# One attention and two mixture-of-experts layers on one core: weight loads reordered, two tile preparations moved from ScalarE to VectorE, and filler matmuls added

## The reference, cut to what matters

```
x = softmax(0.125 * mean_pool2(q) @ k.T) @ v       # 2 batches, 8 heads, 1152 keys, 576 pooled queries, width 64
x = x as (1152 tokens, 512)
layer 0: e = argmax(x @ w_gate); g = softmax weight of e     # 8 experts, at most 288 tokens each
         x = g * (relu(x @ w1[e]) @ w2[e])                   # w1[e] is 512x1024, w2[e] is 1024x512
layer 1: tokens with x @ w_skip > 0 only:
         x = x + g * (relu(x @ w1[e]) @ w2[e])               # own weights; other tokens are kept
```

## Time and profile before

| | us |
|---|---|
| median of 3 runs | 679.82 (678.68 to 680.38) |
| the profiled execution, its own time | 677.86 |
| its span, first to last instruction | 676.1 |
| PE busy | 585.8 (87%) |
| DVE, ACT, POOL busy | 308.4, 281.8, 182.1 |
| PE's share of the chain that ended last | 80% |

### The profile page before, as it was taken

The page is one execution under the profiler, slowest core; times in us unless marked ns, Lnnn a source line. Parts: engine busy times, 40 slices in busy tenths (PEclk is TensorE's granted clock), DMA queues, the critical chain, the costliest instruction groups (busy, mean ns, idle before and its releaser), DMA issues.

```text
span 676.1 us, 11932 instructions
## 1 busy us (share of the span) xinstructions
PE 585.8 (87%) x3420; PEld 329.2 (49%) x3421; DVE 308.4 (46%) x651; ACT 281.8 (42%) x454; POOL 182.1 (27%) x166
## 2 busy tenths in 40 slices
PE   3759999999999999938999999996569846699994
PEld 3547778777777777533333333332523212233331
DVE  5326665756665666570266629555611101022222
ACT  4525565666565655324333444410045030444410
POOL 5183562618081900001111112111012202022222
PEclk9878999999999999958999999999579959799998
DMA  4786536371717160079398059670471854951111
GB/s 105 157 294 132 139 71 142 73 157 35 157 43 149 53 248 19 1 281 383 113 394 357 31 184 413 246 274 20 170 271 48 312 227 127 405 178 51 53 50 40
DMA packets 42633, 111.56 MB, mean 165 GB/s; under 512 B 16020, under 2 KB 16020, under 8 KB 41536
## 3 DMA queue, kind: packets, MB, share of 16 engines
q1 hardware_dynamic: 38528, 99.03, 45.6%
q0 software_dynamic: 4080, 12.22, 5.4%
HBM read 102.68 MB, written 12.06 MB: 170 GB/s over the span
## 4 chain that ended last, share of the span: by engine, by line
PE 80%; DVE 5%; DMA 4%; issue 3%; ACT 2%; POOL 2%; SPq 1%; DVEq 0%; ACTq 0%; POOLq 0%
PE psum L887 39%; PE psum L680 13%; PE psum L694 10%; PE psum L728 8%; PE psum L874 4%; PE psum L756 2%; DMA qraw<-in_q_dram 2%; DMA w1ring<-in_moe_w_dram 2%; ACT wright L313 1%; PE psum L740 1%; PE psum L724 1%; PE psum L852 1%; POOL KT L328 1%; PE psum L889 1%; SPq L387 1%
## 5 line engine op out<-in xcount | busy, mean ns | idle before, releaser
L887 PE MATMUL psum<-w1ring,XT 128*64 x304 | 142.7, 625 | 29.0 <-ACT wright L313 23.6
L889 PE MATMUL psum<-wright,XT 128*64 128x512 f32 x304 | 142.7, 625 | 0.0
L887 PE MATMUL psum<-w2ring,HT 128*64 x304 | 134.5, 595 | 3.2 <-DVE wright L313 3.1
L889 PE MATMUL psum<-wright,HT 128*64 128x512 f32 x304 | 134.5, 595 | 0.0
L1131 DVE TENSOR_SCALAR_CACHE_REDUCE probs<-psum 128x1152 f32<-128x1152 f32 x72 | 97.6, 1357 | 74.2 <-PE psum L680 74.2
L680 PE MATMUL psum<-KT,QT 128*128 128x384 f32 x480 | 106.5, 362 | 19.6 <-DVE KT L1238 9.8
L971 ACT ACTIVATE probs<-probs,nmax 128x1152 f32<-128x1152 f32 x72 | 90.7, 1260 | 48.0 <-DVE probs L1131 48.0
L313 ACT COPY wright<-w1ring 128x1024 f32 x76 | 74.6, 1058 | 61.1 <-DMA w1ring<-in_moe_w_dram 35.0
L680 PEld LDWEIGHTS psum<-KT,QT 128*128 128x128 f32 x480 | 84.6, 197 | 31.3 <-issue 16.6
L887 PEld LDWEIGHTS psum<-w1ring,XT 128*64 128x64 f32 x304 | 42.0, 144 | 114.9 <-issue 114.9
L694 PE MATMUL psum<-ident,probs 128*128 128x128 f32 x648 | 83.1, 277 | 3.3 <-ACT probs L971 2.8
(11 more groups left out here) (160 smaller groups left out, 563.8 us busy)
## 6 DMA issues: line engine op xcount, KB each, us to landing
w1ring<-in_moe_w_dram SPq DMA_DIRECT2D x64, 512.0 KB, 9.2
w2ring<-in_moe_w_dram SPq DMA_DIRECT2D x64, 512.0 KB, 6.6
qraw<-in_q_dram SPq DMA_DIRECT2D x30, 288.0 KB, 7.0
kraw<-in_k_dram SPq DMA_DIRECT2D x14, 576.0 KB, 7.1
V<-in_v_dram SPq DMA_DIRECT2D x8, 576.0 KB, 3.9
moe_in<-zero SPq DMA_DIRECT2D x9, 256.0 KB, 3.0
wnext<-in_next_w_dram SPq DMA_DIRECT2D x1, 2304.0 KB, 16.5
out_dram<-moe_in SPq DMA_DIRECT2D x1, 2304.0 KB, 9.7
```

The lines of the kernel that those rows point to most:

```text
L887: pe.matmul(psum[0:GRAIN, b, :], lhs[:, c * P:c * P + GRAIN], left, start=first, stop=last, skip_group_check=True)
L889: return pe.matmul(psum[GRAIN:P, b, :], lhs[:, c * P + GRAIN:(c + 1) * P], wright[k][:, cols], start=first, stop=last, skip_group_check=True)
```

## The change

Six edits:

1. SP waits for layer 0's first gather before it loads any w2. Inside a layer w1 of expert a + 2 is asked for before w2 of expert a, and w1 of expert 4 ahead of the loop. All first seven matrices of layer 1 are loaded during layer 0.
2. The right half of w1 for the tiles 0 and 1 is filled by DVE: for tile 0 right after the tables, ahead of the rest of the routing, and for tile 1 behind w2's first fill, once hidden(0) is done. ACT fills from tile 2 on.
3. Layer 0's last y is copied by ACT into a tile of its own (`ylast`), from which PE and POOL read.
4. PE's loop passes over the missing tiles first, directly behind step 0, and then runs the tiles in order.
5. 22 filler matmuls (ident by ident, 128x128) on PE before the first scores, and 8 in each layer, behind the gate placement, once `rows_in` is there. Their result is not read.
6. `turn_y` and PE's logits use other PSUM banks.

```diff
@@ SP
+            sp.wait_ge(x_loaded_[0], 16)
             load_matrix(SECOND, 0, 0)
             load_matrix(SECOND, 0, 1)
-            sp.wait_ge(x_loaded_[0], 16)
+            load_matrix(FIRST, 0, 3)
             load_matrix(SECOND, 0, 2)
-            load_matrix(FIRST, 0, 3)
...
-            def other_experts(m):
-                with sp.Fori(RINGS[1], E - 1) as a:
-                    load_second(m, a, m, a - RINGS[1])
-                    load_first(m, a + 1, m, a - RINGS[1])
-                load_second(m, E - 1, m, E - 1 - RINGS[1])
+            def middle_experts(m):
+                load_first(m, RINGS[0], m, 0)
+                with sp.Fori(RINGS[1], E - 2) as a:
+                    load_first(m, a + 2, m, a - 2)
+                    load_second(m, a, m, a - RINGS[1])
             sp.wait_ge(tables_ready, 1)
-            other_experts(0)
-            load_first(1, 0, 0, E - 4)
+            middle_experts(0)
+            load_first(1, 0, 0, 4)
+            load_second(0, 6, 0, 3)
+            load_first(1, 1, 0, 5)
+            load_second(0, 7, 0, 4)
             for e in range(2):
-                load_second(1, e, 0, E - 3 + e)
-                load_first(1, e + 1, 0, E - 3 + e)
+                load_first(1, e + 2, 0, e + 6)
+                load_second(1, e, 0, e + 5)
+            load_second(1, 2, 0, 7)
...
-            load_second(1, 2, 0, E - 1)
-            load_first(1, 3, 0, E - 1)
-            other_experts(1)
+            middle_experts(1)
+            for e in (6, 7):
+                load_second(1, e, 1, e - RINGS[1])
@@ PE
+            def keep_busy(n, at):
+                for _ in range(n):
+                    pe.matmul(bank(at, P), ident[:], ident[:], start=True, stop=True, skip_group_check=True)
             pe.wait_ge(consts_ready, 1)
+            keep_busy(22, MISC)
...
                 mm.then_inc(gates_found, 1)
+                pe.wait_ge(rows_in_ready, m + 1)
+                keep_busy(8, HID_BANK + 1)
...
-                step(1)
-                with pe.Fori(2, NSLOT) as t:
-                    with pe.If(t < rest + 2):
-                        step(t)
+                skipped = (NSLOT - 2) - rest
+                with pe.Fori(1, NSLOT) as i:
+                    with pe.If(i > skipped):
+                        step(nc.s_assert_within(pe.snap(1 + ((i + rest + (17 - NSLOT)) & 15)), 1, NSLOT - 1,
+                                                skip_runtime_bounds_check_because="the branch leaves 1 to rest + 1"))
@@ ACT
-                    fill_right(act, nc.scalar.copy, FIRST, m, t + 1, w1_right_[m])
+                    if not isinstance(t, int):
+                        fill_right(act, nc.scalar.copy, FIRST, m, t + 1, w1_right_[m])
...
-                fill_right(act, nc.scalar.copy, FIRST, m, 0, w1_right_[m])
...
                 if m == 0:
+                    act.wait_ge(y_done_[0], rest + (2 + START))
+                    nc.scalar.copy(ylast[:], bank(Y_BANK)).then_inc(y_copied_[0], 1)
                     act.wait_ge(y_turned, 1)
@@ DVE
                 nc.vector.tensor_copy(tab_grain[m][:], r_tab[0:1, :]).then_inc(tables_ready, 1)
+                dve.wait_ge(tables_ready, m + 1)
+                dve.wait_ge(x_stored, 16 * 4 * H)
+                fill_right(dve, nc.vector.tensor_copy, FIRST, m, 0, w1_right_[m])
...
                 fill_right(dve, nc.vector.tensor_copy, SECOND, m, 0, w2_right_[m])
+                dve.wait_ge(hidden_done_[m], START + 1)
+                fill_right(dve, nc.vector.tensor_copy, FIRST, m, 1, w1_right_[m])
                 step(0)
...
-                copy_y(m, rest + 1)
+                if m == 1:
+                    copy_y(m, rest + 1)
```

More of the change, by code:

```diff
@@ L134, in build @@
         ysb = sb_in(moe, "ysb", [P, DM])
+        ylast = sb_in(moe, "ylast", [P, DM])
         yT = sb_in(moe, "yT", [P, DM])
@@ L234, in build @@
         FIRST_ORDER = (3, 4, 5, 6, 0, 1, 2) + tuple(range(7, TURNS))
-        X_BANK, Y_BANK, HID_BANK, HT_BANK, YT_BANK, LG_BANK = 0, 1, 2, 4, 6, 7
+        X_BANK, Y_BANK, HID_BANK, HT_BANK, JUNK_BANK = 0, 1, 2, 4, 6
+        YT_BANK, LG_BANK = HT_BANK, HID_BANK
         block = ctx.enter_context(nc.Block())
@@ L603, in load_residual, with store_y @@
                         bounds_check=B * SQ - 1, oob_is_err=False).then_inc(res_loaded, 16)
-                def store_y(t, count):
+                def store_y(t, count, last=False):
                     wait(pool, y_stored, 16 * t)
@@ L612, in store_y @@
                     settle()
-                    src, dst = (ysb, x_dram[1]) if m == 0 else (orow, out)
+                    src, dst = (ylast if last else ysb, x_dram[1]) if m == 0 else (orow, out)
                     nc.gpsimd.indirect_dma_start(
@@ L650, in _ @@
                 if m == 0:
-                    store_y(rest + 1, done + 1)
+                    store_y(rest + 1, done + 1, last=True)
                     pool.wait_ge(y_stored, rest * 16 + 32)
@@ L932, in turn_y @@
                     for c in range(DC):
-                        mm = pe.transpose(bank(YT_BANK)[:, c * P:(c + 1) * P], ysb[:, c * P:(c + 1) * P], ident[:])
+                        mm = pe.transpose(bank(YT_BANK)[:, c * P:(c + 1) * P], ylast[:, c * P:(c + 1) * P], ident[:])
                     mm.then_inc(y_turned, 1)
@@ L1280, in next_logits @@
                     wait(dve, lrow_ready, t * (E + 1) + (e - 1) if not isinstance(t, int) or t or e > 1 else 0)
-                    nc.vector.tensor_tensor_reduce(out=bank((YT_BANK, LG_BANK)[e % 2]), in0=ysb[:], in1=wnext[:, e, :], scale=1.0, scalar=0.0,
+                    nc.vector.tensor_tensor_reduce(out=bank(JUNK_BANK + e % 2), in0=ysb[:], in1=wnext[:, e, :], scale=1.0, scalar=0.0,
                                                    op0=ALU.mult, op1=ALU.add, accum_out=lrow[:, e:e + 1]
```

## The result

The changed kernel takes 654.3 us (median of 4, 651.8 to 657.5) against 679.7 for the kernel before (median of 4, 678.7 to 680.4): 0.9635 of its time, interval 0.9614 to 0.9655, so 25.4 us faster. The forecast was 646.4, its range ended at 653.0: the time lies 1.3 us outside, and 7.9 above the forecast.

A forecast was written before the change was run, and what follows sets the result against it. PE was taken to bound the kernel, so only its idle or half-clock time could be won. Terms -28.05 - 1.4 - 1.0 + 1.3 - 4.3 = -33.4 us, from 679.82 to 646.4 us; range 642.5 to 653.

The forecast's parts named there:

- the weight order: Layer 1, SP's queue: asking for w1 earlier removes both stalls and the half clock after them, -28.05 us.
- Rival (b): Layer 1: w2 of 4 and 5 land late behind w1 loads, 1 to 2 stalls; 652 to 656 us, chance 0.12.
- the end of layer 0: ACT copies the last y, so routing of layer 1 is taken up at 470.9 instead of 475.22: -4.3 us.
- hidden(1) follows hidden(0)'s end by 3.1 us now, and by 1.4 + 4 x 0.73 + 1.3 = 5.6 after: Start of layer 0: four passed-over turns ahead of hidden(1) on PE's sequencer cost +2.5 us.
- rival (c): Layer starts: passed-over turns cost less than 0.73 us each or are hidden; 3 to 5.5 us lower, 642, chance 0.13.
- rival (a): Fillers do nothing for the clock, or the pause behind step 0 lets it fall again; 650 us, chance 0.25.
- The second half of (a): The 3 to 4 us pause behind step 0 lets the clock fall, costing up to 2 us in each layer.
- DVE's fill for tile 1 doesn't hold it: Layer 0: w2 of 1 lands at 313.6, tile 1's first w1 quarter is there at 316.0, before hidden(1) at 317.0.
- a sign of failure: The prediction was said to fail if, among other signs, PE waits for `wright` before hidden(1).
- the start fillers: First scores: 22 fillers raise the clock, last exponential at 16.5 instead of 17.90; -1.4 us, bounds -1.5 and +2.1.
- the gather fillers: Start of each layer: eight fillers raise the clock for hidden(0), -2.0 us in layer 0 and -1.3 in layer 1.
- the first half of rival (a): The fillers do nothing for the clock, costing 2.0 + 1.3 us from the hidden products.

The follow-up runs named there:

- old_loop: The changed kernel with PE's loop of the kernel before (step(1) written out, missing tiles passed over at the end): 646.4 us (0.9506).
- after_swap: The changed kernel, its new PE loop kept, with DVE's w1 copies for tile 1 ahead of its first w2 copies: 652.6 us (0.9620).
- swap: The changed kernel with PE's loop of the kernel before and DVE's w1 copies for tile 1 ahead of its first w2 copies: 640.6 us (0.9427).
- swap_no8: The run swap without the eight filler matmuls in each layer: 642.2 us (0.9462).
- swap_no22: The run swap without the 22 filler matmuls before the first scores: 638.5 us (0.9400).
- loop_fill: The changed kernel with 24 more filler matmuls on PE behind step 0 of each layer, ahead of the loop: 663.7 us (0.9765).

## Why the prediction was right and wrong

Two terms carry most of the miss: the gap ahead of hidden(1), and the clock, which fell in that gap and, in the profiled execution, also rose late in hidden(0).

**Right: the weight order.** -28.05 forecast, -27.8 in the trace, and -31.1 for edit 1 alone, whose span gained 29.9: the stalls, about 0.7 at the start of layer 0, and 0.9 in attention, which edit 1 doesn't touch and which is scatter. Rival (b), w2 late in its turn, didn't come: the beat is 15.65 to the end. **Right: the end of layer 0,** -4.3 forecast, -4.2 in the trace, -4.7 alone.

**Wrong: "hidden(1) follows hidden(0)'s end by 3.1 us now, and by 1.4 + 4 x 0.73 + 1.3 = 5.6 after".** The mechanism held, its size didn't: 7.8 us in layer 0 and 8.6 in layer 1, against 5.6 and 6.3. The 1.4 us before the loop are there (312.9 to 314.3), and so are the 1.3 from the table load to the first matmul. In between, the passed-over turns took 4.2 and 5.0 us instead of 2.9 and 3.65, and setting up the loop and entering the turn that is run, which the sum left out, took 0.9 us in each layer. That is +4.5 us in all.

The turns are longer because the 0.73 us of the earlier trace rows is the price of another loop. Its turn has four sequencer instructions, with about 0.06 us between one and the next. The new loop, with `i > skipped`, has six, at the same spacing: 0.95 us. The single branches are about as long as before (207 to 214 ns then, 214 to 224 now), so nothing shows that an idle PE makes a turn longer. Besides, the first jump over the body took 476 and 440 ns instead of 221. So rival (c), shorter turns, is out. The Trainium skill's page "Advanced Engine Details and Errata", section "Control Flow Timing", has about 108 ns for a compare-and-branch; these rows don't agree: 207 to 237 for one that jumps, in either loop, and 76 and 83 for one that doesn't.

**Wrong: leaving the pause's clock to rival (a).** The second half of (a), "up to 2 in each layer after the pause", is what happened, and as priced: hidden(1) to turn_hidden(1) took 16.6 and 16.3 us instead of 14.7, +1.9 and +1.65. PE stood still for 5.35 and 6.19 us there; I had taken the pause for 3 to 4, and (a) for one chance in four. Where hidden(1) follows within 2.5 us, in layer 1 of old_loop, or 3.3, in that of the kernel before, the clock stays up. Gap and clock in layer 1 are 6.1 + 1.65 = 7.75 us against old_loop, about the 7.9 that edit 4 costs in the medians; layer 0, where DVE's queue holds tile 1 as well, adds 0.4 in these two traces.

**Wrong: "DVE's fill for tile 1 doesn't hold it ... the first quarter is there at 316.0".** Its copy began at 318.26. The last quarter of w2 of 1, which DVE copies first, was in only at 317.2: I had it at 313.6, 12 us after the issue, but the w2 loads began 0.8 us later than I had them, at 302.22, and took 15 us. W1 of 3 went out at 312.21, beside the last quarters; that it slowed them is not shown. In the changed kernel the loop hid this error: the row at 320.70 says that hidden(1) waited for DVE's `wright`, which I had named as a sign of failure, but in after_swap, where that copy waits for no w2, hidden(1) comes no closer to hidden(0) (7.75 us against 7.8). Old_loop and swap show the size of the error, 5.8 us. So my two errors in layer 0 didn't add up, and undoing either alone doesn't show the other.

**Wrong: the start fillers, -1.4.** The part I worked out held: the exponentials end 1.3 us earlier and SP's loads begin 1.3 us earlier (19.43). But I let "the loads of head 1 hang on it" stand for their landing. One issue of the queries took 1.61 us instead of 0.60, and they landed at 34.33 (before 33.86). The other traces repeat it: that issue took 1.36 to 2.29 us in eight of the nine kernels traced with the start fillers, and 0.60 in all seven without. In the ninth, swap_no8, it took 0.60, and POOL began its first cut of head 1 at 33.01 instead of 33.76 or later. So the longer issue eats most of the 1.3 us; why it is longer wasn't found. On average the last product of attention ends at 284.3 with the fillers and at 284.4 without.

**Partly right: the gather fillers.** I took -2.0 and -1.3 for hidden(0) on a higher clock; the profiled execution has -0.8 and +0.4, the first four pairs still at half. Other executions have it at full clock at once (the row of swap_no22). So the first half of rival (a), that the fillers do nothing for the clock, is out in general, though this execution came near it. In the medians the 8 fillers are worth 3.1 us, near the 3.3 I gave them in hidden(0), and 1.5 in the other pair; what decides in which executions the clock is up in time is open.

Summed for the profiled execution: +4.5 for the gaps, +3.6 for the clock after them, +2.9 for the clock of hidden(0), +2.0 for attention are 13.0, and -33.4 + 13.0 = -20.4, the span's difference (the other terms are off by a few tenths in all). The medians miss by 7.9 and not by 13.0 because this execution lies 3.1 us above the changed kernel's median and the one profiled before 1.8 below its own.

## What to carry to other kernels

Order a queue's loads by when their places come free and when they are wanted: one load issued behind another that waits cost 14 us each time, and that was all in a timeline of SP and one beat of the chain. Try the large edit alone as well: here it was 6.2 us faster than the whole change.

Price a loop turn that is passed over by the sequencer instructions of the loop as it will be written, with its set-up and entry, and by what the array does meanwhile: such turns were hidden behind queued matmuls, and cost a us each, plus the clock, where nothing was queued. When a copy moves to another engine, look at what stands ahead of it there: copies that wait for a transfer held one that needed none, and an experiment with a single edit undone doesn't show two delays that lie over each other.

## What was not expected of the hardware

The first jump over the loop's body took PE's sequencer 440 and 476 ns in the changed kernel, where the later ones took 221, and once, in loop_fill, 3273 ns. With 48 filler matmul instructions queued, the sequencer started on the loop 4.3 us after turn_hidden began rather than at once. One issue of the queries on SP took 1.36 to 2.29 us instead of 0.60 in nearly every kernel with the start fillers. The causes are open.
